# A three-stage token and channel mixer: transfers of 127 rows split into 112 and 15, and the odd output blocks stored tile by tile

## The chip, the cores and the metric

The kernel runs on one core of a Trainium2 chip. Five engines work side by side, each through its own list of instructions: TensorE (PE in the rows; PEld is its weight load), VectorE (DVE), ScalarE (ACT), GpSimd (POOL) and SyncE (SP), which here does nothing but issue DMA transfers and wait. A transfer is carried out by up to 16 DMA engines, which all issuers share, and it raises its semaphore by 16 when it has landed. The metric is the device time of one execution in microseconds, as the median of several runs: 1015.53 us before the change (three runs, 1014.71 to 1015.89).

## The reference

The input of every stage has 4 batches, 768 tokens and 320 channels (8 heads of 40). Three stages follow on each other.

```python
# stage 1, a recurrence over 768 tokens for each batch and head, state 40 x 40
y[t]  = r[t] @ state
state = state * w[t] - outer(state @ a[t], b[t]) + outer(v[t], k[t])
# stage 2, on x = y as (batch, token, 320)
mixed = real(fft(fft(x, axis=1), axis=2))
u  = x + mixed
un = (u - mean(u)) / sqrt(var(u) + 1e-6)
x  = u + maximum(un @ w_ch1, 0) @ w_ch2          # 320 -> 1280 -> 320
# stage 3
u   = x + (maximum(x.T @ w_tok1, 0) @ w_tok2).T   # 768 -> 256 -> 768 over tokens
out = u + maximum(u @ w_ch1', 0) @ w_ch2'         # 320 -> 1536 -> 320
```

All of it is in single precision; the matrix products are made from high and low parts, so that most products stand three times in the code.

## The kernel before, in words

The program has five parts, one after the other, with a barrier of all engines between them: `attention` (0 to 372 us of the profiled execution), `fourier` (the two FFTs as products with tables, 372 to 457 us), `mlp` "c" (the first channel product), `token_mix`, and `mlp` "d" (the second channel product, which writes the output).

A 128-row tile puts one token in each of the 128 partitions. The activations stay on the chip in `u_all`, 24 tiles of 128 x 320, six to a batch. The first three tiles of a batch hold tokens 0 to 383 in order. The last three hold the upper half in an order that fits the symmetry of the Fourier transform: tokens 385 to 512, then 513 to 640, then 641 to 767 in partitions 0 to 126, and token 384 in partition 127. `upper(rows)` (lines 776 to 782) lists these pieces: two of 128 rows, one of 127 rows, one of a single row. Three places use the list:

- `load_upper` in `fourier` (line 926) loads the upper half of a batch from the attention's output in DRAM into `u_all`. SP issues it for batches 0 and 1 at the start of the part, and for batches 2 and 3 behind `load_halves` of the same batch, which is one transfer of 384 rows into `second` (line 920) and one into `u_all` (line 911). `load_halves` of batch b waits until VectorE has made the first addition of batch b - 2 (`added`, line 1066).
- `token_jobs` loads the token weights in the same order of rows (line 801, one job of 127 + 1 rows) for the splits that GpSimd makes.
- the stores of `mlp` "d" (line 1379) write the upper half of a batch.

In `fourier` each batch b is worked off in the same order: TensorE makes six products of the first stage (line 1200), ScalarE copies each into its high part (`f_g_hi`) and VectorE makes the low part (`f_g_lo`, `f_g_last`, lines 1123 and 1125). Between the low parts of products 0 and 2 VectorE makes the sums and differences of the next batch, `fold` (line 969), which waits for both transfers of `load_halves` of that batch. VectorE works through its list in order, so a late transfer also holds back the low parts behind the fold, and TensorE waits for these. Then come `f_fold_lo` of the next batch (line 996), and the additions of the second stage (`ADD`), in front of which VectorE waits for `upper_in`, the transfers of `load_upper`. GpSimd meanwhile fetches and splits the weights of `mlp` "c" (lines 823 and 827).

In `mlp` "d" a loop runs over eight blocks k of three tiles. TensorE makes the hidden layer (line 1494) and then, tile by tile, the output products (line 1508). VectorE adds each finished tile to `u_all` and writes it to `d_o` (line 1461), which raises `y_done` by one. `d_o` has two halves, one for even and one for odd blocks, and before VectorE writes the first tile of a block it waits for the stores of the block two earlier. SP waits for all three tiles of block k (`TB * k + 2 * TB`, where TB is 3 and the count starts at 3) and then issues one store for an even block (the lower half of a batch) or the four stores of `upper` for an odd one. The last block, k = 7, is odd. At the end SP waits for all stores (line 1384).

Of the kernel before, what the change touches and what calls it, by code (L numbers as in the profile page):

```python
# [11 lines left out]
B, H, S, D = 4, 8, 768, 40  # L12
E = H * D
P = 128
# [730 lines left out]
TB = 3  # L745
# [3 lines left out]
KF = [(0, P), (P, P), (2 * P, E - 2 * P)]  # L749
KR = E - 2 * P  # L750
EPS = 1e-6
STORES = (16, 16 * (1 + S // 2 // P))
PARTS_AT = (0, 2, 6, 7, 9)
PIECE = 320

# [20 lines left out]
def upper(rows):  # L776


    half = S // 2
    n = half // P  # L780
    return [(slice(0, P), j, rows[half + 1 + j * P:half + 1 + j * P + P]) for j in range(n - 1)] + \
           [(slice(0, P - 1), n - 1, rows[S - P + 1:S]), (slice(P - 1, P), n - 1, rows[half:half + 1])]


class Prefetch:
# [65 lines left out]
def token_jobs(w, w1, w2):  # L851

    M = w1.shape[1]
    half = S // 2
    HT = half // P
    out = [(HT * M, [(0, w1[0:half].rearrange("(t p) m -> p t m", p=P))],
            [(w.w1_hi[:, 0:HT, :].rearrange("p c m -> p (c m)"), w.w1_lo[:, 0:HT, :].rearrange("p c m -> p (c m)"), P, slice(0, HT * M))])]
    pieces = upper(w1)
    for t in range(HT):
        srcs = [(rows.start, src) for rows, tile, src in pieces if tile == t]  # L860
        out.append((M, srcs, [(w.w1_hi[:, HT + t, :], w.w1_lo[:, HT + t, :], P, slice(0, M))]))
    for m in range(M // P):
        parts = []
        for slots, cols in ((slice(0, half), slice(0, half)), (slice(half, S - 1), slice(half + 1, S)), (slice(S - 1, S), slice(half, half + 1))):
            parts.append((w.w2_hi[:, m, slots], w.w2_lo[:, m, slots], P, cols))
        out.append((S, [(0, w2[m * P:m * P + P, :])], parts))
    return out
# [8 lines left out]
class FourierInputs:  # L876
# [46 lines left out]
    def load_upper(self, sp, b):  # L923
        HT, x = S // 2 // P, self.x_dram[b]
        for rows, t, src in upper(x):
            sp.dma_start(self.u[rows, NI * b + HT + t, :], src).then_inc(self.upper_in[b % 2], 16)
# [73 lines left out]
def fourier(nc, given, early, norm, start, u, w_jobs):  # L1000
# [4 lines left out]
    with ExitStack() as ctx:  # L1005
# [3 lines left out]
        def sem(name):  # L1009
            return ctx.enter_context(nc.semaphore("f_" + name))  # L1010

        HS = S // 2
        HT = HS // P
# [16 lines left out]
        hi_done = sem("hi_done")  # L1030
        lo_done = sem("lo_done")
        added = sem("added")
        UPPER = 16 * (1 + HT)
        N1 = 6
        MATS = 4
        START_BANKS = (0, 1, 6)
# [77 lines left out]
        def _(dve):  # L1114
            def batch(b):
# [18 lines left out]
                if b < B - 1:  # L1134
                    for eo in (0, 1):
                        early.fold_rest(dve, b + 1, eo)
                dve.wait_ge(upper_in[b % 2], UPPER * (b // 2) + UPPER)

# [189 lines left out]
def mlp(nc, name, ident, u, w, hidden, norm, start, out_dram, stage, next_jobs, last_work):  # L1328


    with ExitStack() as ctx:
# [3 lines left out]
        def sem(n):  # L1335
            return ctx.enter_context(nc.semaphore(f"{name}_{n}"))
# [19 lines left out]
        y_done = sem("y_done")  # L1356
# [11 lines left out]
        @block.sync  # L1368
        def _(sp):
            if prefetch:  # L1370
                prefetch.fetch_all(sp)
            if out_dram is not None:
                sp.sem_inc(stored[0], 1)
                sp.sem_inc(stored[1], 1)
                for k in range(NBLK):
                    sp.wait_ge(y_done, TB * k + 2 * TB)
                    if k % 2:
                        for rows, t, dst in upper(out_dram[k // 2]):
                            sp.dma_start(dst, o[rows, 1, t, :]).then_inc(stored[1], 16)
                    else:  # L1380
                        dst = out_dram[k // 2][0:TW].rearrange("(t p) e -> p t e", p=P)
                        sp.dma_start(dst, o[:, 0, :, :]).then_inc(stored[0], 16)
                for par in (0, 1):
                    sp.wait_ge(stored[par], NBLK // 2 * STORES[par] + 1)

# [35 lines left out]
        def _(dve):  # L1421
# [24 lines left out]
            def main(k, par, j, beside):  # L1446
# [5 lines left out]
                for t in range(TB):  # L1452
# [4 lines left out]
                    else:  # L1457
                        dst = o[:, par, t, :]
                        if t == 0:
                            dve.wait_ge(stored[par], STORES[par] * j + 1)  # L1460
                    nc.vector.tensor_tensor(dst, bank[4 + t % 2][:, 0:E], src, ALU.add).then_inc(y_done, 1)  # L1461
# [290 lines left out]
```

## Time and profile before

| | before |
|---|---|
| median of three runs | 1015.53 us |
| the profiled execution's own time | 1013.78 us |
| its span in the trace | 1011.8 us |
| TensorE busy | 958.3 us, 95% of the span |
| VectorE busy | 500.4 us, 49% |
| ScalarE, GpSimd busy | 349.0 us, 301.7 us |
| mean granted TensorE clock | 0.988 of full speed |

The span goes from the first to the last record of the core, and the profiled execution's own time is 2.0 us longer. TensorE's busy time is modelled from the starts of pipelined matmuls, so that 95% does not say how well it is used, but its gaps are real. An idle VectorE, ScalarE or GpSimd costs nothing by itself.

### The profile page before, as it was taken

The page shows a single profiled execution, that of the slowest core. Times are in us where ns is not written, and L with a number is a line of the kernel's source. Part 1 is how long each engine was busy: PE and PEld are TensorE (multiplying, and loading weights), DVE is VectorE, ACT ScalarE, POOL GpSimd, SP SyncE. Part 2 cuts the span into 40 slices and gives each one's busy share as a digit, 9 for nine tenths or more (in the row PEclk, how much of TensorE's full clock was granted, in tenths as well). Part 3 has the DMA queues.
Part 4 walks back from the last instruction along what each step waited for, and adds up shares of the span by engine and source line. Part 5 has one row for each costly group of instructions (what it writes and reads, how often), then busy time and mean ns, then how long its engine had stood idle before and what let it go on. Part 6 is the DMA issues. An engine that isn't in the chain of part 4 may idle for free. (4 is left out here: it accounts for less than half of the span.)

```text
span 1011.8 us, 48583 instructions
## 1 busy us (share of the span) xinstructions
PE 958.3 (95%) x21467; PEld 911.6 (90%) x21468; DVE 500.4 (49%) x941; ACT 349.0 (34%) x758; POOL 301.7 (30%) x361
## 2 busy tenths in 40 slices
PE   6899999999999679998999999999999999999995
PEld 4788988888888568888999999999999999999995
DVE  4366677766767356765444333346733223322330
ACT  3466666665665433332221111232322112211220
POOL 6456655565566417705200000027500000000000
PEclk9999999999999999999999999999999999999998
DMA  7256666676665344302000000003100000000000
GB/s 250 101 185 210 196 198 202 196 229 209 199 211 174 96 122 156 102 1 68 25 0 0 0 0 0 0 0 107 37 1 20 20 0 19 19 19 6 13 19 19
DMA packets 50249, 86.80 MB, mean 86 GB/s; under 512 B 6066, under 2 KB 29746, under 8 KB 50194
## 3 DMA queue, kind: packets, MB, share of 16 engines
q1 hardware_dynamic: 48578, 81.96, 25.5%
q0 software_dynamic: 880, 3.69, 1.2%
q8 instruction: 28, 0.46, 0.2%
q10 hardware_dynamic: 736, 0.48, 0.2%
q14 instruction: 27, 0.22, 0.1%
HBM read 70.37 MB, written 7.86 MB: 77 GB/s over the span
## 5 line engine op out<-in xcount | busy, mean ns | idle before, releaser
L1412 ACT ACTIVATE d_h_hi<-d_bank 128x384 fp32r<-128x384 f32 x96 | 47.1, 491 | 200.1 <-PE d_bank L1494 200.1
L1449 DVE SCALAR_TENSOR_TENSOR d_h_lo<-d_bank,d_h_hi 128x384 fp32r<-128x384 f32 x96 | 53.5, 558 | 78.1 <-ACT d_h_hi L1412 78.1
L1508 PE MATMUL d_bank<-w_lo,d_h_hi 128*128 128x320 f32 x288 | 89.0, 309 | 0.0
L1508 PE MATMUL d_bank<-w_hi,d_h_lo 128*128 128x320 f32 x288 | 89.0, 309 | 0.0
L1508 PE MATMUL d_bank<-w_hi,d_h_hi 128*128 128x320 f32 x288 | 89.0, 309 | 0.0
L1412 ACT ACTIVATE c_h_hi<-c_bank 128x384 fp32r<-128x384 f32 x80 | 37.5, 489 | 146.4 <-PE c_bank L1494 146.4
L1508 PE MATMUL c_bank<-w_hi,c_h_hi 128*128 128x320 f32 x240 | 74.8, 312 | 0.0
L1508 PE MATMUL c_bank<-w_hi,c_h_lo 128*128 128x320 f32 x240 | 74.1, 309 | 0.0
L1508 PE MATMUL c_bank<-w_lo,c_h_hi 128*128 128x320 f32 x240 | 74.1, 309 | 0.0
L1461 DVE TENSOR_TENSOR d_o<-d_bank,u_all 128x320 f32<-128x320 f32 x24 | 11.8, 492 | 111.0 <-PE d_bank L1508 111.0
L1449 DVE SCALAR_TENSOR_TENSOR c_h_lo<-c_bank,c_h_hi 128x384 fp32r<-128x384 f32 x80 | 42.3, 554 | 40.9 <-ACT c_h_hi L1412 40.9
L1529 POOL TENSOR_TENSOR t_x_lo<-u_all,t_x_hi 128x320 fp32r<-128x320 f32 x6 | 5.1, 883 | 181.3 <-ACT t_x_hi L1524 181.3
L1461 DVE TENSOR_TENSOR u_all<-c_bank,u_all 128x320 f32 x24 | 11.8, 492 | 87.4 <-PE c_bank L1508 87.4
L1508 PEld LDWEIGHTS d_bank<-w_hi,d_h_lo 128*128 128x128 f32 x288 | 54.1, 188 | 0.0
L1508 PEld LDWEIGHTS d_bank<-w_hi,d_h_hi 128*128 128x128 f32 x288 | 54.1, 188 | 0.0
L1508 PEld LDWEIGHTS d_bank<-w_lo,d_h_hi 128*128 128x128 f32 x288 | 54.1, 188 | 0.0
L477 PE MATMUL pr<-du,t_neg 64*64 64x40 f32 x2400 | 52.3, 230 | 1.8 <-issue 0.9
L1494 PE MATMUL d_bank<-fold_hi,w_hi 128*128 128x384 f32 x192 | 50.9, 347 | 2.2 <-DVEq L1464 2.2
L477 PEld LDWEIGHTS pr<-du,t_neg 64*64 64x64 f32 x2400 | 44.6, 137 | 6.3 <-issue 6.3
L395 DVE TENSOR_TENSOR_SCAN suff<-e_raw,restart 128x520 f32<-128x520 f32 x24 | 29.8, 1242 | 37.6 <-POOL spare L261 37.3
L1508 PEld LDWEIGHTS c_bank<-w_lo,c_h_hi 128*128 128x128 f32 x240 | 45.1, 188 | 0.0
L1508 PEld LDWEIGHTS c_bank<-w_hi,c_h_hi 128*128 128x128 f32 x240 | 45.1, 188 | 0.0
(265 smaller groups left out, 2792.1 us busy)
## 6 DMA issues: line engine op xcount, KB each, us to landing
e_raw<-in_e SPq DMA_DIRECT2D x72, 256.0 KB, 4.3
r_raw<-in_c SPq DMA_DIRECT2D x24, 768.0 KB, 4.3
tok<-tok_of SPq DMA_DIRECT2D x24, 320.0 KB, 2.7
e_raw<-in_e SPq DMA_DIRECT2D x24, 260.5 KB, 4.1
va<-in_c SPq DMA_DIRECT2D x24, 160.0 KB, 2.5
vb<-in_c SPq DMA_DIRECT2D x24, 160.0 KB, 2.7
attention_out<-yout SPq DMA_DIRECT2D x92, 40.0 KB, 2.0
stage<-in_moe_w_ch POOLq DMA_DIRECT2D x4, 640.0 KB, 6.9
```

What stands on the lines that cost most here:

```text
L395: nc.vector.tensor_tensor_scan(out[:, ::-1], w_of(n)[:, 1:][:, ::-1], restart[:, 1:][:, ::-1], 1.0, ALU.mult, ALU.add).then_inc(done["suff ...
L477: return nc.tensor.matmul(out, lhs, rhs, start=start, stop=stop, skip_group_check=True)
L1412: nc.scalar.activation(h_hi[:, m, :], bank[m % 4][:, 0:TW], ACT.Relu).then_inc(h_hi_done, 1)
L1449: nc.vector.scalar_tensor_tensor(h_lo[:, m, :], bank[m % 4][:, 0:TW], 0.0, h_hi[:, m, :].bitcast(F32), ALU.max, ALU.subtract).then_inc(h_l ...
L1461: nc.vector.tensor_tensor(dst, bank[4 + t % 2][:, 0:E], src, ALU.add).then_inc(y_done, 1)
L1494: last = nc.tensor.matmul(bank[m % 4][:, 0:TW], lhs, rhs, start=(i == 0), stop=(i == len(parts) - 1))
L1508: last = nc.tensor.matmul(bank[4 + t % 2][:, 0:E], lhs, rhs, start=(m == 0 and i == 0), stop=(m == NM - 1 and i == 2))
L1529: self.nc.gpsimd.tensor_tensor(self.x_lo[:, t, :], self.u[:, t, :], self.x_hi[:, t, :].bitcast(F32), ALU.subtract).then_inc(self.xl_done, 1)
```

## The change

`upper` lists five pieces instead of four: the one of 127 rows becomes 112 rows and 15 rows. The counts that wait for the pieces go up by one transfer (`STORES`, `UPPER`; the job of the token weights counts its own). In the stores of odd blocks SP waits for each tile by itself: for tile t of block k until `y_done` is at `TB * k + TB + t + 1`. The even blocks are stored as before.

```diff
+EVEN = P - 16
-STORES = (16, 16 * (1 + S // 2 // P))
+STORES = (16, 16 * (2 + S // 2 // P))
 ...
     return [(slice(0, P), j, rows[half + 1 + j * P:half + 1 + j * P + P]) for j in range(n - 1)] + \
-           [(slice(0, P - 1), n - 1, rows[S - P + 1:S]), (slice(P - 1, P), n - 1, rows[half:half + 1])]
+           [(slice(0, EVEN), n - 1, rows[S - P + 1:S - P + 1 + EVEN]), (slice(EVEN, P - 1), n - 1, rows[S - P + 1 + EVEN:S]),
+            (slice(P - 1, P), n - 1, rows[half:half + 1])]
 ...
-        UPPER = 16 * (1 + HT)
+        UPPER = 16 * (2 + HT)
 ...
                 for k in range(NBLK):
-                    sp.wait_ge(y_done, TB * k + 2 * TB)
                     if k % 2:
                         for rows, t, dst in upper(out_dram[k // 2]):
+                            sp.wait_ge(y_done, TB * k + TB + t + 1)
                             sp.dma_start(dst, o[rows, 1, t, :]).then_inc(stored[1], 16)
                     else:
+                        sp.wait_ge(y_done, TB * k + 2 * TB)
                         dst = out_dram[k // 2][0:TW].rearrange("(t p) e -> p t e", p=P)
                         sp.dma_start(dst, o[:, 0, :, :]).then_inc(stored[0], 16)
```

Only the lists of SP differ; the other engines keep their instructions and their order, with new line numbers. Here is SP's list at the start of `fourier` before the change. The first eight transfers fill the upper tiles of batches 0 and 1, and the two behind them are `load_halves` of batch 2.

```order
L926 DMA u_all<-attention_out 128x320 x2
L926 DMA u_all<-attention_out 127x320
L926 DMA u_all<-attention_out 1x320
L926 DMA u_all<-attention_out 128x320 x2
L926 DMA u_all<-attention_out 127x320
L926 DMA u_all<-attention_out 1x320
L920 DMA second<-attention_out 128x3x320 [waits f_added,rest_stored,stored1]
L911 DMA u_all<-attention_out 128x3x320
```

The same place after the change:

```order
L928 DMA u_all<-attention_out 128x320 x2
L928 DMA u_all<-attention_out 112x320
L928 DMA u_all<-attention_out 15x320
L928 DMA u_all<-attention_out 1x320
L928 DMA u_all<-attention_out 128x320 x2
L928 DMA u_all<-attention_out 112x320
L928 DMA u_all<-attention_out 15x320
L928 DMA u_all<-attention_out 1x320
L922 DMA second<-attention_out 128x3x320 [waits f_added,rest_stored,stored1]
L913 DMA u_all<-attention_out 128x3x320
```

Ten transfers stand where eight stood, the order is the same, and `load_halves` stands behind them all as before.

The second place is the end of the program, SP's stores of the last two blocks of `mlp` "d", before the change:

```order
L1382 DMA out<-d_o 128x3x320 [waits d_y_done]
L1379 DMA out<-d_o 128x320 [waits d_y_done]
L1379 DMA out<-d_o 128x320
L1379 DMA out<-d_o 127x320
L1379 DMA out<-d_o 1x320
L1331 UNCONDITIONAL_BRANCH [waits d_stored1,d_stored0]
```

And after it:

```order
L1385 DMA out<-d_o 128x3x320 [waits d_y_done]
L1381 DMA out<-d_o 128x320 [waits d_y_done] x2
L1381 DMA out<-d_o 112x320 [waits d_y_done]
L1381 DMA out<-d_o 15x320 [waits d_y_done]
L1381 DMA out<-d_o 1x320 [waits d_y_done]
L1333 UNCONDITIONAL_BRANCH [waits d_stored1,d_stored0]
```

Every store of the odd block has a wait of its own; those of the two whole tiles can be met one and two tiles before the block is complete, while the last three stores wait for the same, third tile.

## Rows read from the trace of the kernel before

**Rows 1.** The page, busy time of each engine: us, share of the span, instructions.
```profile
PE 958.3 (95%) x21467; PEld 911.6 (90%) x21468; DVE 500.4 (49%) x941; ACT 349.0 (34%) x758; POOL 301.7 (30%) x361
```
**Rows 2.** Timeline of DVE at the end: start us, us, engine, line, idle before and releaser.
```profile
995.73 0.49 DVE L1461 TENSOR_TENSOR d_o<-d_bank,u_all 128x320 f32<-128x320 f32 x1 [4.80 <-PE d_bank L1508]
1001.01 0.49 DVE L1461 TENSOR_TENSOR d_o<-d_bank,u_all 128x320 f32<-128x320 f32 x1 [4.79 <-PE d_bank L1508]
```
**Rows 3.** Timeline and waits of SP's queue at the end.
```profile
1001.53 3.45 SPq L1379 DMA_DIRECT2D out<-d_o  x4
SPq L1384 <- DMA out<-d_o: 6.3, 1, 6.3
```
**Rows 4.** Windows after the last addition: stretch, length, busy by engine, PEclk, DMA share, GB/s.
```profile
1001.50:1002.30 0.80, 0.00 (x0) 0.00 (x0) 0.01 (x1) 0.00 (x0) 0.00 (x0) 1.00 0.00 0
1002.30:1003.40 1.10, 0.00 (x0) 0.00 (x0) 0.00 (x0) 0.00 (x0) 0.00 (x0) 1.00 0.84 296
1003.40:1004.20 0.80, 0.00 (x0) 0.00 (x0) 0.00 (x0) 0.00 (x0) 0.00 (x0) 1.00 0.07 10
1004.20:1010.80 6.60, 0.00 (x0) 0.00 (x0) 0.00 (x0) 0.00 (x0) 0.00 (x0) 0.55 0.07 24
1010.80:1011.76 0.96, 0.00 (x0) 0.00 (x0) 0.00 (x0) 0.00 (x0) 0.00 (x0) 0.50 0.00 0
```
**Rows 5.** Transfers by line: ns of issue min/median/max, first and last start; then us to landing.
```profile
L1379 SPq DMA_DIRECT2D out<-d_o x16: 302/392/2339, 800.6 to 1002.8; - x16
DMA to landing us min/median/max: 2.8/2.8/3.0
L175 SPq DMA_DIRECT2D attention_out<-yout x92: 446/597/1452, 62.3 to 370.1; - x92
DMA to landing us min/median/max: 1.8/2.0/3.9
```
**Rows 6.** Windows of the three Fourier periods, from one first low part to the next.
```profile
376.24:394.86 18.62, 18.62 (x113) 16.58 (x111) 13.97 (x25) 6.09 (x11) 11.46 (x17) 1.00 0.61 197
394.86:417.29 22.43, 20.29 (x118) 17.36 (x117) 15.99 (x24) 6.11 (x11) 20.85 (x29) 1.00 0.48 152
417.29:436.86 19.57, 19.57 (x118) 17.54 (x117) 14.22 (x25) 6.09 (x11) 6.11 (x7) 1.00 0.02 8
```
**Rows 7.** Waits of PE, 387 to 412 us: us in total, times, longest.
```profile
PE f_bank L1200 <- DVE f_g_lo L1123: 1.1, 1, 1.1
PE f_bank L1208 <- DVE f_diff L1153: 0.6, 1, 0.6
PE f_bank L1230 <- DVE f_g_last L1125: 0.4, 1, 0.4
```
**Rows 8.** Timeline of DVE around the late fold.
```profile
387.07 0.49 DVE L1150 TENSOR_TENSOR f_diff<-f_bank,f_q 128x320 f32<-128x320 f32 x1 [0.26 <-DMA u_all<-attention_out]
394.86 0.55 DVE L1123 TENSOR_TENSOR f_g_lo<-f_bank,f_g_hi 128x386 fp32r<-128x386 f32 x1
399.84 1.41 DVE L969 TENSOR_TENSOR f_fold<-u_all,second 128x960 f32<-128x960 f32 x1 [4.44 <-DMA u_all<-attention_out]
```
**Rows 9.** Timeline of SP's queue in `fourier`.
```profile
372.82 14.68 SPq L926 DMA_DIRECT2D u_all<-attention_out  x8
387.65 0.39 SPq L920 DMA_DIRECT2D second<-attention_out  x1
388.08 1.13 SPq L911 DMA_DIRECT2D u_all<-attention_out  x1
```
**Rows 10.** Windows: all DMA traffic of two stretches of `fourier`.
```profile
382.50:387.50 5.00, 5.00 (x34) 4.20 (x32) 3.64 (x4) 2.70 (x4) 3.47 (x4) 1.00 0.07 26
396.50:398.50 2.00, 2.00 (x14) 1.81 (x12) 0.00 (x0) 0.53 (x2) 1.70 (x3) 1.00 0.06 24
```
**Rows 11.** Line 911 (`load_lower`), four transfers of 480 KB: us to landing.
```profile
DMA to landing us min/median/max: 3.9/4.7/11.7
```
**Rows 12.** Line 996 in the periods that start at 376.2, 394.86 and 417.29: busy, mean ns, idle.
```profile
L996 DVE TENSOR_TENSOR f_fold_lo<-f_fold,fold_hi 128x960 fp32r<-128x960 f32 x2 | 2.7, 1368 | 0.3 <-ACT fold_hi L992 0.3
L996 DVE TENSOR_TENSOR f_fold_lo<-f_fold,fold_hi 128x960 fp32r<-128x960 f32 x2 | 4.6, 2330 | 0.0
L996 DVE TENSOR_TENSOR f_fold_lo<-f_fold,fold_hi 128x960 fp32r<-128x960 f32 x2 | 2.2, 1155 | 0.3 <-ACT fold_hi L992 0.3
```
**Rows 13.** Timeline of POOL: first weights of `mlp` "c", then the 127-row job of the token weights.
```profile
384.03 3.50 POOL L823 CAST w_hi<-stage 128x320 fp32r<-128x320 f32 x4 [5.95 <-DMA stage<-in_moe_w_ch]
472.66 0.40 POOL L823 CAST tw_hi<-stage 128x256 fp32r<-128x256 f32 x1 [5.62 <-DMA stage<-in_moe_w_tok]
```
**Rows 14.** The page: POOL's last wait in `mlp` "c".
```profile
L1529 POOL TENSOR_TENSOR t_x_lo<-u_all,t_x_hi 128x320 fp32r<-128x320 f32 x6 | 5.1, 883 | 181.3 <-ACT t_x_hi L1524 181.3
```

## The prediction

> **What bounds the kernel now.** I read the page first: TensorE is busy for 958.3 of 1011.8 us [rows 1], so a change of transfers can only earn what lies in TensorE's gaps and behind its last matmul. The two places to look at are therefore the end of the program and the waits of TensorE in the part that uses `upper`.
>
> At the end, the timeline of VectorE gives the last addition: it starts at 1001.01 and lasts 0.49, so all arithmetic is over at 1001.50 [rows 2]. The span is 1011.76. The last 10.26 us are the stores of the last odd block. SP issues four of them from 1001.53 on, taking 3.45 us, and then waits 6.3 us for the landing, to 1001.53 + 3.45 + 6.3 = 1011.28 [rows 3]; 0.48 us of closing work is left. The windows show what the DMA engines do in that time [rows 4]: nothing for 0.8 us; then 1.1 us at a share of 0.84 and 296 GB/s, which is the two whole tiles (2 x 160 KB = 328 kB, and 296 GB/s x 1.1 us = 326 kB); then, after a pause, 6.6 us at a share of 0.07 and 24 GB/s. 0.07 is about 1/16, and 24 GB/s x 6.6 us = 158 kB is nearly the 127 rows x 1280 B = 163 kB. So the piece of 127 rows goes over one DMA engine out of 16, at 6.6 / 127 = 0.052 us for a row.
>
> In `fourier` I compare the periods between the first low parts of successive batches [rows 6]: 18.62, 22.43 and 19.57 us. In the first and third TensorE is busy throughout, in the second it is busy for 20.29 us, 2.14 us less than the period. The waits of TensorE name VectorE's products: 1.1, 0.6 and 0.4 us, 2.1 in all [rows 7]. The timeline of VectorE says why it is late: its fold of batch 2 stood 4.44 us until the lower half of batch 2 had landed, at 399.84 [rows 8]. That transfer was issued at 388.08 [rows 9] and took 11.7 us to land, the longest of four whose median is 4.7 and shortest 3.9 [rows 11]. In 382.5 to 387.5 and again in 396.5 to 398.5 all DMA engines of the core together move 24 to 26 GB/s at a share of 0.06 or 0.07 [rows 10], the same sign of one engine as at the end. SP's eight issues of the upper tiles of batches 0 and 1 take 14.68 us instead of about 8 x 0.4 [rows 5, 9]. I read this so: the two pieces of 127 rows stand in the line of one DMA engine, and the share that this engine has of batch 2's transfers stands behind them.
>
> **The change part by part.**
>
> *Stores of the whole tiles.* Tile 0 and 1 of block 7 are issued as VectorE finishes them; the second at 995.73 + 0.49 = 996.22 [rows 2]. A 480 KB store lands in 2.8 us [rows 5], so both have landed by 999.1, beside TensorE's work on tile 2. This takes two issues, some 0.82 us at the median of 0.392 us and small gaps [rows 5], and their 1.1 us of traffic off the path. The same happens in blocks 1, 3 and 5, where it is worth nothing, as VectorE needs the half of `d_o` again two blocks later. The waits added on SP hold nobody: what is queued behind them are stores that need a later tile anyway.
>
> *The piece of 127 rows.* After 1001.50 SP issues 112 rows, 15 rows and one row, at 1001.53, 1001.95 and 1002.4 (steps of 0.42, as 0.392 with a gap). The first data comes 0.8 us after the first issue [rows 4]. 112 rows over 16 engines are 7 rows each, 7 x 0.052 = 0.36 us; they are through at 1002.7. The 15 rows then take between 0.05 us (one row on each of 15 engines) and 15 x 0.052 = 0.78 us (one engine); no row of this trace shows such a transfer. I take 0.05, since the third issue ends the chain then; at worst the end moves by about 0.4, as 0.78 from 1002.75 ends at 1003.5 and the last row would start at 1003.2. The single row is issued at 1002.4, and the nearest rows are the 40 KB stores of the attention, which land 1.8 us after issue at the least and 2.0 at the median [rows 5]: landed at 1004.2 to 1004.4. With the 0.48 us of closing work the span ends at 1004.7 to 1004.9. From the other side, by traffic: 1002.4 + 0.8 + 0.05 = 1003.25, and the 0.96 us from the last byte to the end [rows 4] give 1004.2. Against 1011.76 this is a gain of 6.9 to 7.6 us. I take 7.1, by the landing of the 40 KB stores, the nearest row.
>
> The Trainium skill, "DMA: Bandwidth & Descriptors", section "Why a DMA increments its semaphore by 16 and not by 1", says that the number of DMA engines is the largest one up to 16 that divides the outer sizes of both sides, so that 127 partitions get one engine; the trace agrees for 127 with its 0.07 of share. By that rule 112 rows get 16 engines and 15 rows get 15, and the sum is the one above; if the 15 rows went over one engine, the term would be 6.7 instead of 7.1.
>
> *The loads of batches 0 and 1.* The two pieces of 127 rows leave the one engine with 2 x (7 + 1 + 1) rows instead of 2 x 128. What SP issues from 372.82 on is 960 KB; at 300 GB/s that is 3.3 us, and ten issues at 0.42 end near 377. VectorE's wait of 0.26 us for the upper tiles of batch 0 [rows 8] goes; TensorE had no gap there [rows 6], so I price it at 0 (0.26 at most). `load_halves` of batch 2 waits for an addition that ends at 387.56, and is issued where it was, at about 387.4 to 387.65. Nothing is left in front of it. With the shortest and the median landing the lower half is there at 388.08 + 3.9 = 392.0 or + 4.7 = 392.8 [rows 9, 11]. The fold is free to start at 394.86 + 0.55 = 395.4 [rows 8]. So the wait of 4.44 us goes whole, with 2.6 us to spare. What is next there is TensorE itself, as in the third period. The gain is at most 22.43 - 19.57 = 2.86 us [rows 6], and no less than 0 if the landing stays where it is. What speaks for a little less: GpSimd is busy for 20.85 us of this period and 6.11 of the next, and beside it `f_fold_lo` took 2.33 us apiece against 1.16 [rows 6, 12]. In the first period GpSimd was at work for 11.46 us and the pair took 2.7 us, and TensorE had no gap. I take 2.7.
>
> *Other loads.* The upper tiles of batches 2 and 3 have no waiter in the rows. The 127-row job of the token weights held GpSimd for 5.62 us [rows 13], but GpSimd later stands 181.3 us before its next needed work [rows 14]: 0. If that cover were gone, the 5.6 us would count.
>
> Sum: 7.1 + 2.7 = 9.8 us, against the profiled execution's own 1013.78: 1004.0. The median of the runs lies 1.75 us above that execution, so the forecast for the median is 1015.53 - 9.8 = 1005.7.
>
> **The rivals.**
>
> *The Fourier wait stays (A).* The transfers of batch 2 share the DMA engines with the weights that GpSimd fetches. If the weights rather than the backlog hold batch 2 back, the fold starts late as before. Against it: at 396.5 to 398.5 only one engine's worth of traffic is left [rows 10]; the others were done by then. It gives 1015.53 - 7.1 = 1008.4.
>
> *Each transfer pays its whole latency in turn (B).* Three small stores after the last tile would take 3 x 2.0 us [rows 5], landing at 1007.5, with 0.48 to 1008.0, a gain of 3.8; with 2.7 that is 1009.0. Against it: the two whole tiles went through in one burst of 1.1 us [rows 4].
> The Trainium skill, "DMA: Bandwidth & Descriptors", section "Rules for kernel authors", speaks against small transfers: under 64 KB one pays mostly overhead, and they should be joined. By it the 15 rows (19 KB) and the single row are all overhead; this would matter here only if the overheads did not overlap, and then the time is that of this rival.
>
> *The split does not spread (C).* If 112 rows still ran over one engine, 112 x 0.052 = 5.8 us would stand instead of 6.6, and the piece would be issued 0.8 us earlier: a gain of 1.6 us at the end, and about none in `fourier`, so 1013.9, which is no change. Against it: pieces of 64 and of 128 rows do not show such a landing (2.0 and 2.8 us) [rows 5].
>
> *GpSimd moves under VectorE (D), slower than before.* GpSimd's first split waited 5.95 us for its weights, to 384.03 [rows 13], beside the same backlog. By 382.5 only one engine was still moving data [rows 10], so it now starts some 1.5 us earlier, and all its splits move with it under VectorE's folds and low parts, which take up to twice as long beside it [rows 12]. If every one of the 24 or 25 VectorE operations of a period lost 0.5 us, each of the first two periods would be 12 us of VectorE work longer, of which VectorE's own idle time (18.62 - 13.97 and 22.43 - 15.99 = 11.1 us in both [rows 6]) covers half: about 13 us lost against 9.8 won. It decides from about 0.45 us an operation. Against it: GpSimd's work only moves, it does not grow, and in the second period it already covers 93%.
>
> **How the numbers follow.** Forecast 0.77, A 0.12, B 0.03, C 0.05, D 0.03. The three runs lie within 1.2 us of each other, and 0.2% (2.0 us) is about what a measurement can tell from no change. The forecast, A and B are all faster by more than that: 0.92; C is within it: 0.05; D: 0.03. The forecast's own range is 1004.2 to 1007.0: down by the upper ends of both terms (7.6 + 2.86 + 0.26 = 10.7) and half the spread of the runs, up by 6.7 + 2.0. To hold A it goes up to 1008.9.
>
> **What would show it.** Right: VectorE's last addition ending near 998.8 and the span 3.2 us behind it, with no stretch of 0.07 share at the end; landing of line 911 below 6 us; the second Fourier period at 19.6 to 20 us and TensorE without a gap in it; SP's ten issues over in 5 us. Wrong: a DMA share of 0.07 for more than 1 us after the last addition (C or the 15 rows), a fold that still waits for its transfer (A), or VectorE operations that are longer throughout `fourier` (D).

## The result, and the profile after

| | before | changed |
|---|---|---|
| median, first comparison | 1015.12 us (4 runs) | 1002.72 us (4 runs, 1002.02 to 1004.66) |
| ratio of the changed kernel to the one before | | 0.9883, 95% interval 0.9864 to 0.9901 |
| the profiled execution's own time | 1013.78 us | 1002.71 us |
| its span | 1011.8 us | 1000.9 us |
| all executions of the study, mean and standard deviation | 1015.5, 2.5 us (82) | 1004.6, 2.1 us (24) |

The change makes the kernel 1.2% faster in the first comparison. Three later comparisons of the same two programs gave 0.9896 (0.9865 to 0.9926), 0.9892 (0.9873 to 0.9911) and 0.9887 (0.9865 to 0.9909). Over all executions, on several chips, the difference of the means is 10.9 us. The forecast was 9.8 us. Differences of 0.2% must not be read from such ratios: the kernel before, run as a program of its own, came out at 0.9983 (0.9968 to 0.9998) of itself.

**The end.** First VectorE's last addition (start, us, engine and line; its idle time and releaser), then the windows behind it (stretch, length, five engines, clock, DMA share, GB/s).

```profile
997.53 0.49 DVE L1464 TENSOR_TENSOR d_o<-d_bank,u_all 128x320 f32<-128x320 f32 x1 [4.79 <-PE d_bank L1511]
```
```profile
998.02:998.82 0.80, 0.00 (x0) 0.00 (x0) 0.01 (x1) 0.00 (x0) 0.00 (x0) 1.00 0.00 0
998.82:999.70 0.88, 0.00 (x0) 0.00 (x0) 0.00 (x0) 0.00 (x0) 0.00 (x0) 1.00 0.62 186
999.70:1000.88 1.18, 0.00 (x0) 0.00 (x0) 0.00 (x0) 0.00 (x0) 0.00 (x0) 1.00 0.00 0
```

The wait of 0.80 us for the first data is what it was [rows 4]. Then 0.88 us at a share of 0.62 moves the whole third tile (186 GB/s x 0.88 us = 164 kB), and 1.18 us later the program is over: 2.86 us behind the last addition instead of 10.26. The stretch of 6.6 us at a share of 0.07 is gone, so the 112 rows were spread over the engines and the 15 rows did not go over one: issued some 0.4 us behind the 112 rows, these alone would have taken 0.78 us more by the 0.052 us for a row, 1.2 us in all, and here all three pieces are through in 0.88. SP's remaining wait for a landing is short:

```profile
SPq L1387 <- DMA out<-d_o: 0.9, 1, 0.9
```

**The Fourier part.** SP's queue, in order of time, answers to [rows 9]:

```profile
373.15 5.07 SPq L928 DMA_DIRECT2D u_all<-attention_out  x10
388.41 0.39 SPq L922 DMA_DIRECT2D second<-attention_out  x1
388.84 0.49 SPq L913 DMA_DIRECT2D u_all<-attention_out  x1
```

Ten issues take 5.07 us where eight took 14.68, and `load_halves` of batch 2 is issued almost where it was, 11.8 us behind the first low part of the period instead of 11.4. The three periods, from one first low part to the next, answer to [rows 6]:

```profile
376.57:395.56 18.99, 18.88 (x113) 16.51 (x111) 14.55 (x24) 6.10 (x11) 14.19 (x21) 1.00 0.59 177
395.56:415.11 19.55, 19.54 (x118) 17.51 (x117) 14.13 (x25) 6.11 (x11) 16.78 (x25) 1.00 0.63 187
415.11:434.70 19.59, 19.59 (x118) 17.55 (x117) 14.06 (x25) 6.11 (x11) 6.77 (x8) 1.00 0.00 1
```

The second one is 19.55 instead of 22.43 us and TensorE has no gap in it. VectorE's fold of batch 2, which stood 4.44 us [rows 8], starts at once:

```profile
396.17 1.16 DVE L971 TENSOR_TENSOR f_fold<-u_all,second 128x960 f32<-128x960 f32 x1
```

It does so by a hair. The lower half of batch 2 took 7.3 us to land in this trace, the longest of the four transfers of its line, and was there at 388.84 + 7.3 = 396.1:

```profile
DMA to landing us min/median/max: 3.9/4.8/7.3
```

In the other six traces of the changed kernel this landing took 4.5 to 6.7 us, in the five of the kernel before 11.4 to 12.1.

The first period has become 0.37 us longer. GpSimd's first split now starts at 381.70, 2.3 us earlier than in [rows 13], and runs for 14.19 instead of 11.46 us of the period; the pair of `f_fold_lo` in it takes 1.76 us apiece instead of 1.37 [rows 12].

```profile
381.70 1.66 POOL L825 CAST w_hi<-stage 128x320 fp32r<-128x320 f32 x4 [3.29 <-DMA stage<-in_moe_w_ch]
```
```profile
L998 DVE TENSOR_TENSOR f_fold_lo<-f_fold,fold_hi 128x960 fp32r<-128x960 f32 x2 | 3.4, 1756 | 0.3 <-ACT fold_hi L994 0.3
```

**Where the rest is.** End and second period give 7.40 + 2.88 = 10.3 us, while the spans differ by 10.9. To find the rest I cut every trace at the same events: VectorE's first table operation of `fourier` (end of the attention), the four first low parts (the first of them 2.28 or 2.29 us behind the table operation in every trace; this piece is not in the table), SP's first load of `mlp` "c", VectorE's first copy into `second` of `mlp` "d", its last addition, and the end. The 5 traces of the kernel before and the 7 of the changed one, all taken in this study, give these means (lowest to highest), in us:

| stretch | before | changed | difference |
|---|---|---|---|
| attention | 376.1 (373.7 to 380.1) | 375.8 (373.9 to 378.0) | -0.3 |
| first Fourier period | 18.61 (18.60 to 18.62) | 18.81 (18.60 to 19.05) | +0.2 |
| second | 22.31 (20.90 to 22.80) | 19.83 (19.54 to 20.29) | -2.5 |
| third | 19.56 | 19.56 | 0 |
| fourth, to the first load of "c" | 20.66 | 20.66 | 0 |
| `mlp` "c" and `token_mix` | 280.65 (280.59 to 280.86) | 279.46 (277.83 to 280.69) | -1.2 |
| `mlp` "d", to the last addition | 263.39 | 263.39 | 0 |
| end | 10.25 | 2.86 | -7.4 |

The sum is -11.2 us. Three stretches repeat to 0.03 us; most of the spread between the traces lies in the attention, which the change doesn't touch. Behind the third term, 1.2 us, stands TensorE's clock after the gaps between the parts. In the kernel before, the first 2 us of matmuls of each channel product (windows from their first matmul) run partly at the lower of the two levels, 1.2 instead of 2.4 GHz:

```profile
457.91:459.91 2.00, 2.00 (x8) 2.00 (x9) 0.00 (x0) 0.00 (x0) 0.00 (x0) 0.70 0.62 214
731.08:733.08 2.00, 2.00 (x8) 2.00 (x9) 0.00 (x0) 0.00 (x0) 0.00 (x0) 0.67 0.03 8
```

In the first trace of the changed kernel, after the same waits of 2.6 and 2.2 us, the granted clock stays at the upper level in the first case and falls in the second:

```profile
455.69:457.69 2.00, 2.00 (x11) 2.00 (x12) 0.00 (x0) 0.30 (x1) 0.00 (x0) 1.00 0.51 160
727.62:729.62 2.00, 2.00 (x7) 2.00 (x8) 0.00 (x0) 0.00 (x0) 0.00 (x0) 0.58 0.03 8
```

### The profile page after: what moved, and what is told of

Same layout as the page of the kernel before. It is cut to its first block and busy times, and to the rows that moved or that the text cites. A ratio compares the mean times of both kernels' runs of the same rounds, so it can differ in the third digit from the quotient of the medians.

```text
span 1000.9 us, 48593 instructions
## 1 busy us (share of the span) xinstructions
PE 957.8 (96%) x21468; PEld 910.1 (91%) x21468; DVE 498.9 (50%) x941; ACT 349.4 (35%) x758; POOL 301.6 (30%) x361
## 5 line engine op out<-in xcount | busy, mean ns | idle before, releaser
L1464 DVE TENSOR_TENSOR d_o<-d_bank,u_all 128x320 f32<-128x320 f32 x24 | 11.8, 491 | 111.1 <-PE d_bank L1511 111.1
L1464 DVE TENSOR_TENSOR u_all<-c_bank,u_all 128x320 f32 x24 | 11.8, 492 | 87.5 <-PE c_bank L1511 87.5
```

## The experiments

**One half of the change at a time.** The first four kernels ran on one chip. The changed kernel again:

> The changed kernel once more, beside the kernel before. Theory (two terms and the clock): 7.4 us come from the last stores and 2.6 us from the loads in the Fourier part, 10.0 in all, and what was measured beyond that is in which executions TensorE's granted clock falls to its lower level at the gaps between the parts; then the difference of medians moves between 9 and 13 us from one set of runs to another, and the executions with a lower mean clock are the longer ones. Rival (a third term): the change itself saves some 1.3 us at the start of the first channel product, and the difference stays at 11.3 to 12.5 us.

The difference of the medians was 9.6 us, and "c" and `token_mix` took 280.69 us in this trace, as in the kernel before: a term that the change always brings is ruled out. Of the six runs the two shortest had the highest mean clock (999.62 and 1002.74 us at 0.988, the others at 0.983 to 0.985).

Stores alone:

```diff
-def upper(rows):
+def upper(rows, split=False):       # 127 rows in one piece unless asked
 ...
-        UPPER = 16 * (2 + HT)
+        UPPER = 16 * (1 + HT)
 ...
-                        for rows, t, dst in upper(out_dram[k // 2]):
+                        for rows, t, dst in upper(out_dram[k // 2], True):
```

> Only the stores of the output are changed (112 + 15 + 1 rows, each tile with a wait of its own); the loads keep 127 rows. Theory: the stretch from the last addition to the end falls from 10.3 to 2.9 us, everything before it stays, with the fold of batch 2 still waiting some 4.4 us: 7.4 us faster. Rival (a third term that hangs on the loads): the same here, 7.4 us, and the first channel product at half clock for its first 3 us as before.

Loads alone (the pieces of the loads split, `STORES` and the waits of the stores as before; shown against the changed kernel):

```diff
-                            sp.wait_ge(y_done, TB * k + TB + t + 1)
+                    sp.wait_ge(y_done, TB * k + 2 * TB)             # before the loop over the pieces
-                        for rows, t, dst in upper(out_dram[k // 2]):
+                        for rows, t, dst in upper(out_dram[k // 2], False):
```

> Only the loads are changed (attention output and token weights in 112 + 15 + 1 rows); the output is stored as before, in 128, 128, 127 and 1 rows after the third tile. Theory: the second Fourier period falls from 22.4 to 19.6 us, the end stays at 10.3 us: 2.6 us faster, give or take the clock at the gaps (1.7 us each). Rival (a third term from the loads, the clock at the start of the first channel product stays up): 4 us faster. Rival A of the prediction (the fold waits for other traffic): no change.

Only the waits for each tile, with 127 rows in one piece everywhere (`STORES` and `UPPER` have their old counts again):

```diff
-           [(slice(0, EVEN), ...), (slice(EVEN, P - 1), ...),
-            (slice(P - 1, P), n - 1, rows[half:half + 1])]
+           [(slice(0, P - 1), n - 1, rows[S - P + 1:S]), (slice(P - 1, P), n - 1, rows[half:half + 1])]
```

> 127 rows stay in one piece everywhere; only SP's wait for each tile of an odd block is new. Theory: the piece of 127 rows is issued right after the last addition instead of third, 0.84 us earlier, and still takes 6.6 us over one DMA engine: the end stretch is about 9.4 instead of 10.3 us, 0.8 us faster. Rival (the early stores of whole tiles matter by themselves, by freeing the queue): 2 us or more faster.

| kernel | median, us | ratio to before (95%) | second period | "c" and token | end |
|---|---|---|---|---|---|
| before | 1014.77 (23 runs) | | | | |
| changed | 1005.18 (6) | 0.9896 (0.9865 to 0.9926) | 19.56 | 280.69 | 2.86 |
| stores only | 1006.51 (6) | 0.991 (0.9884 to 0.9937) | 23.24 | 280.58 | 2.53 |
| loads only | 1013.58 (12) | 0.9982 (0.9958 to 1.0006) | 20.58 | 280.59 | 10.25 |
| waits only | 1012.51 (12) | 0.9986 (0.9964 to 1.0008) | 21.04 | 280.59 | 9.12 |

The stores alone give the whole end term (2.53 us, with the same 0.88 us of traffic; its closing work was 0.3 us shorter than in the other traces, which nothing here explains) and leave the Fourier period as it was, with the fold waiting as before:

```profile
402.52 1.46 DVE L972 TENSOR_TENSOR f_fold<-u_all,second 128x960 f32<-128x960 f32 x1 [4.79 <-DMA u_all<-attention_out]
```

The loads alone take away the fold's wait, which refutes rival A, and leave the end, with its 6.6 us of one engine. Splitting the load of the token weights is worth nothing, as priced: "c" and token take 280.59 us. The second period is 20.58 and not 19.56 us, since the pair of `f_fold_lo` fell under GpSimd's splits and took 2.10 us apiece; the additions behind it came late, and TensorE waited 0.4 us for `f_diff`:

```profile
1006.87:1013.47 6.60, 0.00 (x0) 0.00 (x0) 0.00 (x0) 0.00 (x0) 0.00 (x0) 0.56 0.07 24
L999 DVE TENSOR_TENSOR f_fold_lo<-f_fold,fold_hi 128x960 fp32r<-128x960 f32 x2 | 4.1, 2096 | 0.3 <-ACT fold_hi L995 0.3
PE f_bank L1211 <- DVE f_diff L1156: 0.4, 1, 0.4
```

The waits alone are worth 1.1 us at the end (0.8 expected). So of the 7.4 us the tile-by-tile waits carry 1.1, which leaves 6.3 for the split. The whole differences of the loads alone and of the waits alone, 1.2 and 2.3 us in the medians, can't be told from nothing by their intervals; the traces show their terms.

**Which split.** 113 and 14 rows are as good as 112 and 15 by size and by number of pieces.

```diff
-EVEN = P - 16
+EVEN = P - 15      # 113 + 14 rows; P - 2 in the other kernel: 126 + 1 rows
```

> The changed kernel with 113 and 14 rows in place of 112 and 15, loads and stores alike. Theory (only pieces whose rows can be dealt out evenly use many engines; 113 is prime): the last stretch has 113 x 0.052 = 5.9 us at a share of 0.07 and is 8.5 us long, the fold of batch 2 waits about 4 us again; some 1.7 us faster than before. Rival (any split helps, since the pieces are smaller or are issued apart): as the changed kernel, about 10 us faster, 2.9 us at the end.

> The changed kernel with 126 and 1 rows in place of 112 and 15. Theory (the rows are dealt out over the largest number of engines, up to 16, that divides them; 126 = 14 x 9): 126 rows over 14 engines, 9 x 0.052 = 0.5 us; end stretch 2.9 to 3.1 us, second Fourier period 19.6 us, as fast as the changed kernel. Rival (only multiples of 16, or powers of two, are spread): the end stretch stays near 9 us, as with 113.

With 113 rows the one-engine stretch is back, 6.03 us at a share of 0.07:

```profile
1003.27:1005.17 1.90, 0.00 (x0) 0.00 (x0) 0.00 (x0) 0.00 (x0) 0.00 (x0) 1.00 0.08 17
1005.17:1011.20 6.03, 0.00 (x0) 0.00 (x0) 0.00 (x0) 0.00 (x0) 0.00 (x0) 0.58 0.07 22
1011.20:1012.10 0.90, 0.00 (x0) 0.00 (x0) 0.00 (x0) 0.00 (x0) 0.00 (x0) 0.50 0.00 0
```

The end is 8.83 us and the kernel 1011.46 us in the median (10 runs; ratio 0.9951, 0.9932 to 0.9971). That is 4.0 us faster than before where 1.7 was expected; the end came out as expected, the Fourier part did not (below). With 126 rows it is spread, over 0.90 us:

```profile
1002.96:1003.86 0.90, 0.00 (x0) 0.00 (x0) 0.00 (x0) 0.00 (x0) 0.00 (x0) 1.00 0.58 182
```

End 2.86, second period 19.55, median 1006.33 us (4 runs; 0.9893, 0.9872 to 0.9914), no different from the changed kernel on that chip (1005.33; 0.9887). So 112 = 16 x 7 and 126 = 14 x 9 rows are spread, while 113 and 127, which are prime, are not. It is not the smaller size, and not that pieces were issued apart. This settles rival C. It agrees from both sides with the rule of the Trainium skill, "DMA: Bandwidth & Descriptors", section "Why a DMA increments its semaphore by 16 and not by 1", that the number of engines is the largest one up to 16 that divides the number of rows; how many engines carried the 112 or the 126 rows was not counted here.

The 113 rows also show how the backlog turns into time. The fold still waited 2.31 us, and yet the second period was 19.80 us:

```profile
402.14 1.16 DVE L971 TENSOR_TENSOR f_fold<-u_all,second 128x960 f32<-128x960 f32 x1 [2.31 <-DMA u_all<-attention_out]
```

What counts is when VectorE is through with the pair of `f_fold_lo` behind the folds. In all 13 traces of the study with a second period above 19.6 us the next first low part comes 7.61 to 7.66 us after the end of the pair; where the pair ends by 11.6 us of the period, the period is 19.54 to 19.56 us. The pair in the kernel before, with 113 rows and in the changed kernel:

```profile
405.09 4.58 DVE L996 TENSOR_TENSOR f_fold_lo<-f_fold,fold_hi 128x960 fp32r<-128x960 f32 x2
408.12 3.31 DVE L998 TENSOR_TENSOR f_fold_lo<-f_fold,fold_hi 128x960 fp32r<-128x960 f32 x2 [0.33 <-ACT fold_hi L994]
404.41 2.48 DVE L998 TENSOR_TENSOR f_fold_lo<-f_fold,fold_hi 128x960 fp32r<-128x960 f32 x2 [0.33 <-ACT fold_hi L994]
```

Counted from the first low part the pair starts at 10.23, 8.85 and 8.85 us. So a fold that is 2.3 us late does not delay the pair; one that is 4.44 us late starts the pair 1.38 us late, and the pair then takes 4.58 instead of 2.48 us. Of these 3.5 us 0.6 are slack, and 2.9 are the difference of the periods. The slow pair is thus the larger part of the delay, and the wait of the fold alone doesn't tell the loss: waits of 4.12, 4.44, 4.47, 4.66 and 4.79 us in the kernel before went with pairs of 3.64, 4.58, 4.58, 4.58 and 4.61 us and periods of 20.90, 22.43, 22.73, 22.80 and 22.71 us. A slow pair also comes without a late fold, as in the loads alone (4.11 us, period 20.58). There and in the kernel before GpSimd's splits run beside the pair; how much of its length is owed to the late fold and how much to the place of the splits no run sets apart.

**The clock at the gaps.** Two kernels get matmuls whose product is never read, behind TensorE's last work of the Fourier part and of the token part:

```diff
                 second(b, SECOND[-2:])
+            for _ in range(11):
+                nc.tensor.matmul(bank[7][:, 0:E], mats[0].hi[:, 0, 0:P], mats[0].hi[:, 0, :], start=True, stop=True, ...)
 ...
                 start.turn(pe, f, bank[START_BANKS[f]])
+            pe.wait_ge(y_done, NI * B + 2)
+            for _ in range(10):
+                nc.tensor.matmul(bank[NM + 1][:, 0:E], w1_hi[:, 0, 0:P], h_hi[:, 0, :], start=True, stop=True, ...)
```

> The changed kernel, with 11 and 10 matmuls of no use (their product is never read) behind TensorE's last work of the Fourier part and of the token part, some 1.6 us each, in a gap in which TensorE otherwise waits for VectorE and the barrier. Theory (the granted clock falls there because TensorE stands idle for 2.6 and 2.2 us): the clock stays up at the start of both channel products, 1.3 us each, 2.6 us faster than the changed kernel. Rival (the clock does not look at these gaps, or the extra matmuls push the barrier out): same or slower by up to 1 us.

> The kernel before with the same idle matmuls. Theory: 2.6 us faster than before, from the first 3 us of each channel product, with the fold of batch 2 and the last 10.3 us as they were. Rival: no change.

The gaps shrink from 2.6 and 2.2 us to 0.9 and 0.7, and the clock stays up at both:

```profile
PE c_bank L1499 <- DVEq L1469: 0.9, 1, 0.9
PE d_bank L1499 <- DVEq L1469: 0.7, 1, 0.7
```
```profile
459.42:461.42 2.00, 2.00 (x11) 2.00 (x12) 0.00 (x0) 0.32 (x1) 0.00 (x0) 1.00 0.52 178
731.01:733.01 2.00, 2.00 (x11) 2.00 (x12) 0.00 (x0) 0.31 (x1) 0.00 (x0) 1.00 0.03 8
```

The stretch "c" and token takes 277.45 us in the changed kernel with this filling and 277.66 in the one before, against 280.6: 3.0 us for two gaps, against 2.6 expected. So the length of this stretch follows the clock, and with the idle time of TensorE cut to 0.9 and 0.7 us the clock did not fall. Whole times can't show it: the kernel before with the filling has the ratio 0.9982 (0.9967 to 0.9997; 1013.61 us, 12 runs, against 1015.46), no other than that of the kernel before against itself, and the changed one 0.9876 (0.9856 to 0.9897; 5 runs), where the changed one without it had 0.9892.

**Does the third term belong to the change?** The changed kernel was measured a third and a fourth time, and the kernel before as a run of its own:

> The changed kernel a third time. Theory (two terms, the rest is spread between executions): the mean difference stays at about 10 us, and the first channel product takes 280.6 us from its first load to the last part's first copy, its first 3 us at half clock, as in five of six traces so far. Rival (a third term of 1.3 us there): 279.3 us, as in the first trace of the changed kernel.

> The kernel before, as a run of its own. Theory (two terms, and a third one that falls by chance at the gaps between the parts): end 10.3 us, second Fourier period 21 to 23 us, and 280.6 us for the first channel product and the token part, as in all traces with 127 rows so far, or less by 1.3 or 1.7 us when the clock happens to stay up. Rival (the third term belongs to the change): 280.6 us again.

> The changed kernel a fourth time, for the third term. Theory: as before_again, 280.6 us or less by 1.3 or 1.7; the three traces so far gave 279.3, 280.7 and 278.9. Rival (it belongs to the change): below 280 us again. Both: end 2.9 us, second Fourier period 19.6 us.

The changed kernel had medians of 1004.52 us (0.9892) and 1005.33 us (0.9887), the kernel before 1014.93 us (12 runs). The stretch was 278.87 and 277.83 us in the changed kernel and 280.63 in the one before. So that it would not rest on these, six single executions with a trace followed, three of each:

> The kernel before, one look for the stretch from the first load of the first channel product to the first copy of the last part. Chance: in at least one look of three of this kernel it is shorter than 280.6 us by 1.3 us or more. It belongs to the change: 280.6 us in all three.

> The changed kernel, one look for the same stretch. Chance: 280.6 us in some of three looks. It belongs to the change: under 280 us in at least two of three.

> The kernel before, second look. Chance: under 279.5 us in at least one of three; belongs to the change: 280.6 us in all three.

> The changed kernel, second look. Chance: 280.6 us in some of three; belongs to the change: under 280 us in two of three.

> The kernel before, third look. Chance: under 279.5 us in at least one of three; belongs to the change: 280.6 us in all three.

> The changed kernel, third look. Chance: 280.6 us in some of three; belongs to the change: under 280 us in two of three.

The kernel before gave 280.60, 280.86 and 280.59 us (whole times 1013.39, 1017.92, 1013.72), the changed one 280.61, 278.32 and 280.58 (1004.83, 1004.74, 1007.43). Neither side had its way: the changed kernel was short once in three, where the rival wanted two, and the kernel before never, where chance wanted one. Over all traces the clock stayed up at one or both gaps in 4 of 7 of the changed kernel and in none of 5 of the kernel before, nor in the four with one half of the change or with 113 rows; the one with 126 rows had 280.62. The gaps themselves are the same length. What sets the two cases apart no run here shows, and it stays open whether the change brings it about or it fell that way.

**The filling together with a second queue.** The filling, and for the last block alone the two small pieces issued by ScalarE:

```diff
+                            if k == NBLK - 1 and rows.start >= EVEN:
+                                continue                               # in SP's loop
 ...
+            if out_dram is not None:                                   # at the end of ScalarE's list
+                act.wait_ge(y_done, TB * NBLK + TB)
+                for rows, t, dst in upper(out_dram[B - 1]):
+                    if rows.start >= EVEN:
+                        act.dma_start(dst, o[rows, 1, t, :]).then_inc(stored[1], 16)
```

> The changed kernel with the idle matmuls and, for the last block alone, the pieces of 15 and of 1 row issued by ScalarE's queue while SP issues the 112 rows. Theory (the end is: the last addition, the issue of the last small piece, its landing of about 2 us with the closing work): the last piece is issued 0.4 us earlier, the end stretch falls from 2.86 to 2.45 us; with the clock kept up at both channel products (277.5 us instead of 280.6) it is some 3 us faster than the changed kernel at most. Rival (the 112 rows set the end): 2.86 us stays.

It has the lowest median of the study: 1001.80 us (5 runs), ratio to the kernel before 0.9847 (0.9826 to 0.9868), while the changed kernel had 0.9887 (0.9865 to 0.9909) on the same chip; the two intervals just touch. Its "c" and token stretch is that of the filling (277.65 us). The second queue adds nothing that can be seen: the end is 2.77 us where the seven traces of the changed kernel have about 2.8 to 2.9, and its traffic takes the same 0.88 us at the same place behind the last addition (997.43) as before.

```profile
998.23:999.11 0.88, 0.00 (x0) 0.00 (x0) 0.00 (x0) 0.00 (x0) 0.00 (x0) 1.00 0.63 186
```

The expectation failed. The two small pieces were issued by 0.95 us behind the last addition instead of 1.14, 0.2 us sooner where 0.4 was expected, and the traffic ended 1.68 us behind it as before. The rival, that the 112 rows set the end, fits better, but no run takes the small pieces away to show it alone.

## Why the prediction was wrong

The direction was right, and both mechanisms were found where the prediction had put them; the time, 1002.72 us, lies outside 1004.2 to 1008.9. The step that failed is the one headed "How the numbers follow", in its width and in what it left out. The forecast for the median, 1005.7 us, missed by 3.0 us, in two parts. Over all executions the change is worth 10.9 us and not 9.8: the sum was 1.1 us short, for want of the clock at the gaps, 1.2 us (the end gave 0.3 us more than summed, the second period 0.2 less, the first took 0.2). And the median of the first four runs lay 1.9 us below the mean of all 24 executions of the changed kernel, 1004.6 us. That mean is inside the range, so that the first comparison fell outside is in part the chance of four runs; but the range was there to hold this chance, and it allowed 0.6 us for it.

- **The spread of the executions.** I took the three runs before, within 1.2 us of each other, for the spread of the kernel, and allowed half of that below. Over 82 executions the standard deviation is 2.5 us, from 1009.4 to 1021.7. A difference of two medians of four runs is uncertain by more than 1.5 us from this alone. The first comparison gave 12.4 us, all of them together 10.9; the 1.5 us between are no more than that. The profiled executions, 1013.78 and 1002.71 us, differ by 11.1; the first lies 1.75 us below the median of its three runs, the second on the median of its four.
- **No term for the clock at the gaps.** The prediction summed two terms and put nothing for the start of the channel products, a stretch in which no instruction had changed; 1.2 us on the average came from there, by the granted clock. It was visible in the trace that the clock is low there, so that up to 3 us could come or go. Whether it was owed to the change is open, as told above; that a range should have had room for it is not.
- **The end, 7.1 us: measured 7.4.** The bound by traffic was the better one (7.6). It had the last byte 1.75 us behind the last addition, measured 1.68, and 0.96 us of closing behind that, measured 1.18. The nearest row that I chose, the 40 KB stores of the attention with at least 1.8 us from issue to landing, was too slow for the single row.
- **The Fourier period, 2.7 us: measured 2.9 in the first trace and 2.5 on the average.** The wait of the fold went whole, and the bound of 2.86 us was right, but the sum is right in part by luck. The wait was read as the whole loss; 1.38 us of it came through and the rest was the slow pair of `f_fold_lo` beside GpSimd, which the prediction had as a caveat for 0.16 us. In the four traces of the changed kernel with the shortest periods the pair cost nothing, in the other three 0.6 to 0.7 us. The 2.6 us to spare before the fold were not there either: the landing that was to stay below 6 us took 7.3 us in the first trace and more than 6 in four of seven, and what slowed it no run sets apart.
- **The first period, priced at 0: measured +0.2.** That GpSimd starts earlier under VectorE is the mechanism of rival D, in small: 0.2 us where D needed 9.8. As a reason for a slower kernel it is refuted.
- **Rival A** is refuted by the loads alone, where the fold does not wait; **B** by the 0.88 us of traffic for three pieces; **C** by the changed kernel, while its mechanism, a split that does not spread, is what 113 rows show.
- **Whole tiles and waits.** Stores of tiles 0 and 1 cost nothing, as priced, and taking them from behind the last addition gives 1.1 us by itself. The waits added to SP held nobody up: `mlp` "d" up to its last addition takes 263.39 us with and without them.
- **A slip in the sum.** The upper end of the forecast's own range, 1015.53 - 6.7 - 2.0, is 1006.8 and not 1007.0; nothing hangs on it.

## What to carry to other kernels

Look at the DMA share of every slow transfer: 1/16 for microseconds was here, with 127 and with 113 rows, a transfer whose number of rows has no useful factor. Cutting it into a multiple of 16 and a small rest was worth its extra issue, at the end of the program and where something stood behind it in the queue. A late transfer costs nothing until it uses up the slack of the engine that waits; here a wait of 2.3 us was free and one of 4.4 was not, and the larger part of the delay came from an operation that ran slower behind it. So look for the gap in the bounding engine, and for what ends it, before counting the wait. And before giving a range, ask how far executions of this kernel spread and which stretch of it does the spreading: three runs do not tell.

## What the runs showed that I had not expected

- A transfer over one DMA engine holds its issuer too. With 127 rows SP's eight issues took 14.68 us, the longest single one in `fourier` 10.7 us (up to 11.3 in the other traces of the kernel before), and the issue of a single row behind the 127 at the end took 2.34 us; with 112 and 15 the longest took 1.32 us in the first trace and 2.10 in the worst.
- TensorE's clock fell at idle gaps of 2.2 to 2.6 us in every trace of the kernel before, but not in all of the changed one, and never when useless matmuls had cut them to 0.7 to 0.9 us. Filling the two gaps is worth 3.0 us of the stretch behind them.
- The attention part, with the same instructions in all kernels, took 373.7 to 380.1 us, while `mlp` "d" up to its last addition repeats to 0.02 us. Its spread is as large as most changes that one would try on this kernel, and what sets it stays open: the stretch took 374.9 us in one trace and 380.1 in another at the same granted clock of 0.96.
